# A linear-attention, gated-MLP and soft-routing kernel on one core: the program behind the last tile rewritten

## The reference

```python
# 1: recurrent attention over 768 steps, 4 batches x 8 heads of 48 channels -> x [3072, 384]
# 2: gated MLP
h = x @ w_in; x = (h * np.cos(h)) @ w_out           # d_ff = 2048
# 3: soft routing over 32 slots (8 experts x 4), experts of width 1024
logits = x @ phi                                     # [3072, 32]
d = exp(logits - logits.max(0)); d /= d.sum(0)       # over tokens
slot_input = d.T @ x                                 # [32, 384]
slot_out[e] = np.maximum(slot_input[e] @ w1[e], 0) @ w2[e]
c = exp(logits - logits.max(1)); c /= c.sum(1)       # over slots
out = c @ slot_out
```

## Time and profile before

| | |
|---|---|
| median of 3 runs | 715.07 us (715.0 to 716.31) |
| profiled execution | 714.17 us, of which span 712.4 us |
| PE busy (matmul) | 603.8 us, 85% of the span |
| DVE busy | 504.8 us, 71% |
| ACT busy | 325.8 us, 46% |
| POOL busy | 224.8 us, 32% |
| PE clock granted, mean | 0.963 of full |
| DMA | 81.36 MB, mean 114 GB/s |

### The profile page before, as it was taken

One profiled execution on the slowest core, in us unless ns is written; L12 is line 12 of the kernel. 1 busy time (PEld: TensorE's weight loads), 2 busy tenths in 40 slices (PEclk: granted clock), 3 DMA queues, 4 the chain that ended last, 5 costly groups with the idle time before them and its releaser, 6 DMA issues.

```text
span 712.4 us, 12400 instructions
## 1 busy us (share of the span) xinstructions
PE 603.8 (85%) x4533; PEld 529.0 (74%) x4533; DVE 504.8 (71%) x1268; ACT 325.8 (46%) x713; POOL 224.8 (32%) x194
## 2 busy tenths in 40 slices
PE   2628888889897999899989998899979899995883
PEld 2517778879886988788878887888879889982242
DVE  8827897598759894979588957987697854443313
ACT  1534534534544546354645464446534556462012
POOL 3262553334223422433143324242334222221000
PEclk9967999999999999999999999999999999997797
DMA  9962022310331043104121403122310019864347
GB/s 326 318 218 93 1 62 95 107 51 19 140 106 51 1 156 103 54 2 156 31 84 44 127 33 103 51 73 86 106 50 15 6 25 412 348 214 170 102 164 265
DMA packets 44293, 81.36 MB, mean 114 GB/s; under 512 B 4160, under 2 KB 26816, under 8 KB 44224
## 3 DMA queue, kind: packets, MB, share of 16 engines
q1 hardware_dynamic: 44224, 80.48, 32.9%
HBM read 71.02 MB, written 4.72 MB: 106 GB/s over the span
## 4 chain that ended last, share of the span: by engine, by line
PE 58%; DVE 25%; ACT 8%; issue 5%; SPq 1%; DMA 1%; POOL 0%; DVEq 0%; ACTq 0%; POOLq 0%
PE yb L954 20%; PE hb L939 18%; DVE zs L1121 4%; PE ab L789 3%; DVE ang L1354 3%; PE ab L814 3%; PE ab L808 3%; DVE r_end L1157 3%; DVE ang L1362 2%; DVE A L1197 2%; PE ab L827 2%; PE yb L1063 1%; PE pb L964 1%; DVE tmp L1138 1%; ACT turns L676 1%
## 5 line engine op out<-in xcount | busy, mean ns | idle before, releaser
L556 POOL TENSOR_TENSOR g_lo<-ang,g_hi 128x384 fp32r<-128x384 f32 x128 | 132.0, 1032 | 387.1 <-DVE g_hi L1367 387.1
L939 PE MATMUL hb<-x_hi,win 128*128 128x384 f32 x768 | 221.1, 342 | 33.9 <-DVE ang L1362 21.4
L954 PE MATMUL yb<-wout,g_hi 128*128 128x384 f32 x768 | 207.4, 351 | 2.4 <-POOL g_lo L556 2.4
L939 PEld LDWEIGHTS hb<-x_hi,win 128*128 128x128 f32 x768 | 143.0, 191 | 41.4 <-DVE ang L1362 26.3
L954 PEld LDWEIGHTS yb<-wout,g_hi 128*128 128x128 f32 x768 | 134.4, 190 | 14.1 <-issue 7.2
L682 ACT ACTIVATE ang<-ang 128x384 f32<-128x384 f32 x128 | 67.3, 526 | 169.4 <-DVE ang L1354 169.3
L939 PE MATMUL hb<-x_lo,win 128*128 128x384 f32 x384 | 130.1, 339 | 0.0
L954 PE MATMUL yb<-wout,g_lo 128*128 128x384 f32 x384 | 129.9, 338 | 0.0
L676 ACT ACTIVATE turns<-hb 128x384 int32<-128x384 f32 x128 | 62.7, 490 | 116.2 <-PE hb L939 116.1
L1354 DVE SCALAR_TENSOR_TENSOR ang<-turns,hb 128x384 f32<-128x384 int32 x128 | 70.6, 551 | 61.6 <-ACT turns L676 61.0
L1362 DVE SCALAR_TENSOR_TENSOR ang<-ang,hb 128x384 f32<-128x384 f32 x128 | 69.9, 546 | 46.6 <-ACT ang L684 46.6
(11 more groups left out here) (203 smaller groups left out, 705.3 us busy)
## 6 DMA issues: line engine op xcount, KB each, us to landing
over_att<-w_dram SPq DMA_DIRECT2D x8, 1536.0 KB, 11.9
zs<-zs_dram SPq DMA_DIRECT2D x16, 384.0 KB, 3.4
zp<-zp_dram SPq DMA_DIRECT2D x16, 384.0 KB, 3.8
kT<-k_by_channel_dram SPq DMA_DIRECT2D x16, 384.0 KB, 5.0
rT<-r_by_channel_dram SPq DMA_DIRECT2D x16, 384.0 KB, 6.0
over_win<-w_dram SPq DMA_DIRECT2D x4, 1536.0 KB, 8.6
over_wout<-w_dram SPq DMA_DIRECT2D x4, 1536.0 KB, 7.4
r_tok<-r_by_token_dram SPq DMA_DIRECT2D x16, 288.0 KB, 5.5
```

Source lines behind the costliest of these rows:

```text
L556: g.tensor_tensor(g_lo[f % RING][:, :], ang[f % 2][:, :], g_hi[f % RING][:, :].bitcast(F32), ALU.subtract).then_inc(glo_done, 1)
L939: last = t.matmul(hb[f % 2][:, 0:TT], win[:, f, w, k, :], x[:, k, :], start=(n == 0), stop=(n == 3 * DK - 1))
L954: last = t.matmul(yb[c][:, 0:DM], gx[f % RING][:, c * P:(c + 1) * P], wout[:, f, w, :], start=(f == 0 and n == 0), stop=(f == NF - 1 and n ...
```

## The change

The diff rewrites what follows the last tile's own slots, on every engine; the eight tiles before it are untouched.

- The call of `tile_steps` for the late part is gone. PE first waits for `post_done` of the seventh tile and transposes its and the earlier tiles' combine weights (20 of 24 chunks, in five transposes), and only then runs `mlp_down` of the last two blocks.
- `post` of the last tile is written out by hand over several PSUM banks: `x2` is copied by ACT and DVE, the nine transposes go to three banks, their copies are split over ACT and DVE. The maximum over all chunk rows (`mx_full`, `gm_full`) is worked out while the tile's exponentials run. The exponentials go to a new tile `lE`.
- Combine weights stay in fp32, 32 rows for each chunk, four chunks stacked on 128 rows (`cT`); the three parts and their DVE and PE work are gone. Zeroing `siT` moves to POOL.
- Experts: both groups' first layers run back to back, then the transposes. Relu and copies are split over DVE and ACT.
- The second layer runs by halves of 192 columns, in the order (half 0, g 0), (0, 1), (1, 0), output of half 0, (1, 1), output of half 1. An output matmul has K = 32 and 192 columns in fp32; four chunks take the four row parts of the array. Each copy still moves 384 columns of a row (two chunks). Twelve DMAs of 4 chunks x 192 columns store the result.
- Two w2 parts of group 1 are loaded early, two late.

The diff, cut; declarations of tiles and semaphores, some lines of the softmax on DVE and most removed lines (they stand in the kernel above) are left out:

```diff
+HALF = DM // 2
+PAIRS_OUT = NT * CH // 8
...
+so_rep = sb("so_rep", [P, DM], where=tail)
+cT = sb("cT", [P, NT * CH // 4, P], where=tail)
+over_att = [sb(f"over_att{j}", [P, DK * EF], where=tail) for j in range(6)]
+w2_homes = [HOMES[8:], over_att[4:] + over_att[:2]]
+ob = [HOMES[4 + n][:, :].rearrange("p (a c n) -> p a c n", a=2, n=DM) for n in range(PAIRS_OUT)]
+XT = [pb, hb[0], hb[1]]
+OB = [pb, yb[0], yb[1], yb[2], ab[1], hb[1]]
...
+H1B = [yb[1], yb[2], hb[0], hb[1]]
+H1T_BANKS = [[ab[0], ab[1]], [yb[0], pb]]
...
-    load_w2(1, 0)
+    for j in range(2):
+        load_w2(1, j)
...
-    sp.wait_ge(t_full, 3)
-    for j in range(1, 4):
+    sp.wait_ge(h_exp_full, 2)
+    for j in range(2, 4):
         load_w2(1, j)
-    for n in range(NCT):
-
-        sp.wait_ge(o_act, 2 * (n + 1))
-        sp.wait_ge(o_dve, 2 * (n + 1))
-        sp.dma_start(out_d[n], ob[n][:, :, :]).then_inc(stored, 16)
-    sp.wait_ge(stored, 16 * NCT)
+    for half in range(2):
+        cols = slice(half * HALF, (half + 1) * HALF)
+        for n in range(PAIRS_OUT):
+            sp.wait_ge(o_act, 2 * (half * PAIRS_OUT + n + 1))
+            sp.wait_ge(o_dve, 2 * (half * PAIRS_OUT + n + 1))
+            for m in range(2):
+                sp.dma_start(out_d[2 * n + m][:, :, cols], ob[n][:, m, :, cols]).then_inc(stored, 16)
+    sp.wait_ge(stored, 16 * 4 * PAIRS_OUT)
...
-    pool.wait_ge(post_done, NT)
+    pool.wait_ge(y_step, NT * NF)
+    g.memset(siT[:, :, :, :], 0.0).then_inc(cleared, 1)
     g.memset(pick[:, :, :, :, :], 0.0).then_inc(picked, 1)
...
+    act.wait_ge(ct_full, 1)
+    a.copy(cT[:, 0:4, :], ab[0][:, :].rearrange("p (m n) -> p m n", n=P)).then_inc(ct_read, 1)
+    act.wait_ge(ct_full, 2)
+    a.copy(cT[:, 4:EARLY_CT, :], ab[1][:, 0:(EARLY_CT - 4) * P].rearrange("p (m n) -> p m n", n=P)).then_inc(ct_read, 1)
+    act.wait_ge(y_step, NT * NF)
+    act.wait_ge(pb_full, (NT - 1) * POST_USES)
+    for c in (0, 2):
+        a.activation(x2[:, c, :], yb[c][:, 0:DM], ACT.Copy, scale=-1.0).then_inc(x2_act, 1)
+    for dk in (0, 2):
+        act.wait_ge(xT_full, dk + 1)
+        a.copy(x2T[:, dk, :], XT[dk][:, 0:TT]).then_inc(xT_act, 1)
+    act.wait_ge(max_done, NT)
+    a.activation(alpha[:, :], run_max[:, :], ACT.Exp, bias=neg_max[:, 0:1]).then_inc(exp_done, 1)
+    a.activation(lE[:, :], lT[:, :], ACT.Exp, bias=neg_max[:, 0:1], accum_out=tile_sum[:, :]).then_inc(lE_done, 1)
+    act.wait_ge(gm_done, 1)
+    a.activation(alpha_all[:, :], new_max[:, :], ACT.Exp, bias=neg_all[:, 0:1]).then_inc(alpha_done, 1)
+    act.wait_ge(cdiff_done, 1)
+    a.activation(ctok[:, :, :], ctok[:, :, :], ACT.Exp).then_inc(cexp_done, 1)
+    act.wait_ge(cleared, 1)
+    act.wait_ge(siT_full, 1)
+    a.copy(siT[:, :, :, 0:SPE], yb[0][:, 0:DK * NS].rearrange("p (k e s) -> p k e s", k=DK, e=E)).then_inc(siT_done, 1)
+    act.wait_ge(ct_full, 3)
+    a.copy(cT[:, EARLY_CT, :], ab[1][:, 0:P]).then_inc(ct_read, 1)
+    for g in range(2):
+        act.wait_ge(h_exp_full, 2 * g + 2)
+        a.activation(h1[:, g, 512:EF], H1B[2 * g + 1][:, :], ACT.Relu).then_inc(relu_act, 1)
+        act.wait_ge(h1T_full, 2 * g + 2)
+        a.copy(h1T[:, g, 4:8, :], H1T_BANKS[g][1][:, :].rearrange("p (m n) -> p m n", n=P)).then_inc(h1T_act, 1)
+    def outputs(half):
+        for u in range(0, 4 * PAIRS_OUT, 2):
+            n = half * 4 * PAIRS_OUT + u
             act.wait_ge(o_full, n + 1)
+            a.copy(ob[u // 4][:, :, u % 4, half * HALF:(half + 1) * HALF],
+                   OB[n % 6][:, :].rearrange("p (a n) -> p a n", a=2)[:, :, 0:HALF]).then_inc(o_act, 1)
...
+    def chunks_to_rows(m, bank, at):
+        return t.transpose(bank[:, at * P:(at + 1) * P], c_all[:, 4 * m:4 * m + 4, :].rearrange("p c n -> p (c n)"), ident[:, :])
+    pe.wait_ge(post_done, NT - 1)
+    for m in range(4):
+        last = chunks_to_rows(m, ab[0], m)
+    last.then_inc(ct_full, 1)
+    for m in range(4, EARLY_CT):
+        last = chunks_to_rows(m, ab[1], m - 4)
+    last.then_inc(ct_full, 1)
+    for f in range(NF - LAG, NF):
+        mlp_down(NT - 1, f)
+    pe.wait_ge(g_done, NT * NF)
+    pe.wait_ge(pb_read, (NT - 1) * POST_USES)
+    for c in range(CH):
+        if c == 1:
+            pe.wait_ge(x2_dve, 1)
+        else:
+            pe.wait_ge(x2_act, c // 2 + 1)
+        for dk in range(DK):
+            last = t.transpose(XT[dk][:, c * P:(c + 1) * P], x2[:, c, dk * P:(dk + 1) * P], ident[:, :])
+            if c == CH - 1:
+                last.then_inc(xT_full, 1)
+    for k in range(DK):
+        if k == 1:
+            pe.wait_ge(xT_dve, 1)
+        else:
+            pe.wait_ge(xT_act, k // 2 + 1)
+        for c in range(CH):
+            last = t.matmul(yb[0][NS * c:NS * (c + 1), 0:P], phi[:, k, :], x2T[:, k, c * P:(c + 1) * P],
+                            start=(k == 0), stop=(k == DK - 1), skip_group_check=True)
+    last.then_inc(lg_full, 1)
+    pe.wait_ge(lt_done, 1)
+    t.transpose(yb[1][:, 0:CS], lT[:, :], ident[0:CS, 0:CS]).then_inc(lt_full, 1)
+    pe.wait_ge(max_all, 3)
+    t.matmul(yb[2][0:1, 0:CS], new_max[:, :], ident[0:CS, 0:CS], start=True, stop=True).then_inc(mx_full, 1)
+    pe.wait_ge(mx_row, 2)
+    t.matmul(yb[2][0:CS, 0:1], max_row[:, :, :].rearrange("p c n -> p (c n)"), ones[0:1, 0:1], start=True, stop=True)\
+     .then_inc(gm_full, 1)
+    pe.wait_ge(lE_done, 1)
+    t.transpose(hb[0][:, 0:CS], lE[:, :], ident[0:CS, 0:CS]).then_inc(dt_full, 1)
+    pe.wait_ge(dt_done, 1)
+    for c in range(CH):
+        last = t.matmul(pb[NS * c:NS * (c + 1), 0:DM], dtok[:, c, :], x2[:, c, :], start=True, stop=True)
+    last.then_inc(add_full, 1)
+    pe.wait_ge(merge_done, 1)
+    pe.wait_ge(acc_done, 2)
+    t.matmul(hb[1][0:NS, 0:DM + 1], merge[:, :], acc[:, :], start=True, stop=True).then_inc(si_full, 1)
+    pe.wait_ge(si_done, 1)
     for k in range(DK):
         last = t.transpose(yb[0][:, k * NS:(k + 1) * NS], si[:, k * P:(k + 1) * P], ident[0:NS, 0:NS])
+    last.then_inc(siT_full, 1)
+    pe.wait_ge(siT_done, 1)
+    pe.wait_ge(cdiff_done, 1)
     for g in range(2):
         pe.wait_ge(w1_in[g], 64)
         for half in range(2):
             for k in range(DK):
                 for j in range(4):
+                    last = t.matmul(H1B[2 * g + half][32 * j:32 * j + 32, :], siT[:, k, 4 * g + j, :],
                                     w1[g][j][:, k, half * 512:(half + 1) * 512],
                                     start=(k == 0), stop=(k == DK - 1), skip_group_check=True)
...
+            last.then_inc(h_exp_full, 1)
+        if g == 0:
+            pe.wait_ge(c_last, 1)
+            pe.wait_ge(ct_read, 2)
+            chunks_to_rows(EARLY_CT, ab[1], 0).then_inc(ct_full, 1)
+    pe.wait_ge(ct_read, 3)
...
+    for g in range(2):
         for n in range(2):
+            if n:
+                pe.wait_ge(relu_act, g + 1)
+            else:
+                pe.wait_ge(relu_dve, g + 1)
             for m in range(4):
                 f = n * 4 + m
...
+                last = t.transpose(H1T_BANKS[g][n][:, m * P:(m + 1) * P], h1[:, g, f * P:(f + 1) * P], ident[:, :])
+            last.then_inc(h1T_full, 1)
...
+    def second_layer(half, g):
+        cols = slice(half * HALF, (half + 1) * HALF)
         pe.wait_ge(w2_in[g], 64)
+        pe.wait_ge(h1T_dve, g + 1)
+        pe.wait_ge(h1T_act, g + 1)
         for f in range(EF // P):
             for j in range(4):
+                last = t.matmul(hb[1 - half][32 * j:32 * j + 32, 256 * g:256 * g + HALF], h1T[:, g, f, 32 * j:32 * j + 32],
+                                w2[g][j][:, f, cols], start=(f == 0), stop=(f == EF // P - 1), skip_group_check=True)
+        last.then_inc(so_full, 1)
+    def slots_out(half):
+        cols = slice(half * HALF, (half + 1) * HALF)
+        pe.wait_ge(so4_done, half + 1)
+        pe.wait_ge(picked, 3)
+        for g in range(2):
+            last = t.matmul(ab[0][:, 0:HALF], pick[:, g].rearrange("p r e s -> p (r e s)"), so4[:, g, cols], start=(g == 0), stop=(g == 1))
+        last.then_inc(pick_full, 1)
+    def outputs(half):
+        cols = slice(half * HALF, (half + 1) * HALF)
+        pe.wait_ge(so_done, half + 1)
+        for pair in range(PAIRS_OUT):
+            for m in range(2):
+                for r in range(4):
+                    n = (half * PAIRS_OUT + pair) * 4 + r
+                    if m == 0 and n >= 6:
+                        pe.wait_ge(o_dve if n % 2 else o_act, n // 2 - 2)
+                    rows = slice(32 * r, 32 * r + 32)
+                    last = t.matmul(OB[n % 6][:, 256 * m:256 * m + HALF], cT[rows, 2 * pair + m, :], so_rep[rows, cols],
+                                    start=True, stop=True)
+                    if m == 1:
+                        last.then_inc(o_full, 1)
+    second_layer(0, 0)
+    second_layer(0, 1)
+    second_layer(1, 0)
+    slots_out(0)
+    outputs(0)
+    second_layer(1, 1)
+    slots_out(1)
+    outputs(1)
...
+    dve.wait_ge(y_step, NT * NF)
+    dve.wait_ge(pb_full, (NT - 1) * POST_USES)
```

(84 more changed lines are left out.)

172 lines of the change are left out of this document (68 added, 104 removed).

## The result

| kernel | median | range | runs |
|---|---|---|---|
| before | 715.04 us | 710.95 to 716.31 | 4 |
| after | 706.26 us | 705.44 to 708.85 | 4 |

Paired on the same chip, after takes 0.9896 of the time of before, with a 95% interval of 0.9869 to 0.9923: about 7.4 us less (1.04% of 715); the plain medians differ by 8.8. The forecast was 703.3, so the gain is there and 3 us of it are missing. The plain median lies inside the range of 700.0 to 707.3 and close to the 706.6 of rival 1; by the paired ratio the time of after is 707.6 (0.9896 x 715.04), just above the range.

A forecast was written before the change was run, and what follows sets the result against it. The eight tiles were taken as bound by the MLP's matmuls, followed by 67.2 us with hardly any overlap. The terms summed to -11.75 us: execution 714.17 to 702.4, median 703.3, range 700.0 to 707.3.

The forecast's parts named there:

- rival 1: Clock falls already in the hole before MLP blocks 14 and 15, which run at half speed: 3.1 more, 706.6; chance 0.12.
- F: Output, from the first half's so_rep to the end: stores by column halves at 373 GB/s, 17.7 us for 15.3, +2.3.
- A: End of the MLP: its last two blocks stand behind the wait for post_done and five transposes, a new stall, +2.15 us.
- B: Logits, from the MLP's end: copies split over ACT and DVE, fewer transposes behind the last copy, 2.6 us for 6.3, -3.7.
- C: Softmax and merge, up to the experts' start: the trip for the maxima leaves the path, siT zeroing is hidden, -2.8 us.
- D: Experts' first layers: both groups back to back, then transposes and split copies, 15.3 us for 16.35, -1.0.
- E: Experts' second layer and gather, to the first so_rep: three half-column groups of 2.6 us, one gather, -8.7 from 17.75.
- rival 4: The late w2 loads for the experts' second layer come late, by up to 1 us: 704.3; chance 0.05.
- Rival 3: Output matmuls: the array's row parts do not run side by side, 24.8 us in place of 17.7, 710.4; chance 0.06.
- Rival 2: The clock holds through the softmax, saving time there and 2 us at the experts: 699.7; chance 0.07.
- Rival 5: Last DMAs: short-piece stores at a fraction of the rate, slower than before below 183 GB/s, 718.9 at 160; chance 0.02.

The follow-up runs named there:

- the dense destination: The changed kernel with each column half of the output stored as one dense block, without gaps in HBM: median 705.94 us, 0.9891 of before.

## Why the forecast held in part

The direction and most terms were right; the likeliest time was 3 us too low. Two steps failed: the rate that F took for the stores (373 GB/s, measured 320), and the dismissal of rival 1 in A (the clock fell in the hole and cost 1.5). By its steps:

- **A, the wait: right at +2.15, wrong in what it left out.** The wait alone measures 2.1. What failed is the choice against rival 1, "The rows speak against it so far": I argued from the fall at 649.9, which came late although PE did thin work before it. But that was thin work and this is none. PE stood wholly still for 2.8 us. Nor was 1.2 us the longest hole that kept the full clock: ahead of the tail the trace of before stays at 1.00 behind six holes of 1.9 us and one of 2.17 (it ends at 110.8). None there is as long as 2.8, so no row settled the question. A single trace would not have settled it either: near 217 us that of before keeps 1.00 behind a 1.9 us hole, and that of the dense destination is at 0.51 from 220 to 222. The clock cost 1.5 at the place, half of rival 1's 3.1, because it was back after about 3 us while I let both blocks run slow. Rival 1's mechanism came true in two of three traces; that its 706.6 fits the median is partly chance, since F fills the other half.
- **B: -3.3 for -3.7.** Mis-sized: I counted ACT's two copies (0.9) and three transposes behind them (0.3), so 1.2 to the last transpose. But the nine transposes start only behind the first copy, at 651.22, 0.66 behind the MLP's end, and run 0.11 apart, so the last ends at 1.63 and PE, not ACT, bounds this stretch.

```profile
651.22 0.30 PE L1097 MATMUL pb<-ident,x 128*128 128x128 f32 x1 [0.67 <-ACT x L784]
```

- **C and D: right**, -2.6 for -2.8 and -1.1 for -1.0. The exchanged order of the maxima and the sums costs nothing visible, and ACT's relu asked for no table.
- **E: -8.2 for -8.7.** The groups are as forecast. The margin of 0.7 on the `w2` loads was too small: their traffic ended 10.5 behind the issue in place of 9.9. This is rival 4, at 0.35 (the layer went on at 680.56 instead of 680.21, when PE was ready). The step that failed is "a load of 1.57 MB at 0.4 takes 3.9", read from a kernel with other addresses. The term's own parts also add up to 9.2 and not 9.05, so to -8.55.
- **F: +4.6 for +2.3, the largest miss.** `so_rep` of half 1 came at +8.6, not +7.7: PE left the first outputs 0.75 later than the 3.1 I gave it, since each pair waits for a copy. From there to the end took 11.3, not 10.0: 2.36 MB at 320 take 7.4 instead of 6.3. The 373 I worked out from the earlier trace rows was right for the piece length, as the 372 and 370 of three runs show. The failure is that I took the rate as a property of the length alone and did not follow what three small new tiles do to the addresses. The range's lower bound of 345 GB/s was too high for the same reason. (The term's 17.7 against 15.3 is +2.4, not +2.3.)
- **Rival 3 fell**: four row parts run side by side. One into `pb` and three into `yb` start together, the next four 0.26 later and those after them 0.16 us apart, and the second bank group begins 0.76 after the first (688.02), where 0.7 was forecast:

```profile
687.26 0.42 PE L1189 MATMUL pb<-so_rep,cT 32*128 32x192 f32 x1 [0.45 <-DVE so_rep L1620]
687.27 0.44 PE L1189 MATMUL yb<-so_rep,cT 32*128 32x192 f32 x3
687.53 0.32 PE L1189 MATMUL pb<-so_rep,cT 32*128 32x192 f32 x1
687.69 0.32 PE L1189 MATMUL pb<-so_rep,cT 32*128 32x192 f32 x1
```

- **Rival 2 fell**: the clock is at 0.50 from 656 to 664. **Rival 5 fell**: 320 GB/s is far above 183.

## What to carry to other kernels

Before a block of matmuls is moved behind a wait, look how long PE is then wholly idle: a wait of 2.1 us cost 3.5 to 3.6 at its place in two traces and 2.1 in a third, and doing the blocks first took all of it back. What a clock fall costs is then read over every stage up to its next return, and from more than one trace. And a change that adds a small tile moves every tile behind it: compare the start addresses of the DMA's tiles and the rates of DMAs that the change does not touch.
